# The routing of a fused attention and expert kernel: rounds two to five by order instead of by search

## The reference

```python
for t in range(S):
    state = f[:, :, t, :, None] * state + np.einsum('bhd,bhe->bhde', k[:, :, t], v[:, :, t])
    y[:, :, t] = np.einsum('bhd,bhde->bhe', q[:, :, t], state)
...
logits = x @ w_gate                       # 3072 tokens, 8 experts
order = np.argsort(-logits.flatten())
for idx in order:                         # best pair first
    tok, e = (int(idx) // E, int(idx) % E)
    if assigned[tok] >= 0 or counts[e] >= cap:
        continue
    assigned[tok] = e
    counts[e] += 1
for e in range(E):
    h = np.maximum(x[mask] @ w1[e], 0.0)  # 384 -> 1024
    out[mask] = h @ w2[e]                 # 1024 -> 384
...
h = x @ w_in                              # 384 -> 2048
g = h * np.clip(h + 3.0, 0.0, 6.0) / 6.0
out = g @ w_out                           # 2048 -> 384
```

## Time and profile before

| | us |
|---|---|
| median of 3 runs | 885.61 (885.39 to 890.78) |
| the profiled execution | 886.32 |
| its span | 883.8 |
| busy in it: TensorE, VectorE, ScalarE, GpSimd | 825.5, 384.3, 346.7, 324.8 |
| mean granted clock of TensorE | 0.964 |

### The profile page before, as it was taken

The page is one execution under the profiler, slowest core; times in us unless marked ns, Lnnn a source line. Parts: engine busy times, 40 slices in busy tenths (PEclk is TensorE's granted clock), DMA queues, the critical chain, the costliest instruction groups (busy, mean ns, idle before and its releaser), DMA issues.

```text
span 883.8 us, 15679 instructions
## 1 busy us (share of the span) xinstructions
PE 825.5 (93%) x6030; PEld 795.6 (90%) x6030; DVE 384.3 (43%) x717; ACT 346.7 (39%) x631; POOL 324.8 (37%) x249
## 2 busy tenths in 40 slices
PE   5999999965569999999999999999999999999995
PEld 4899989854459999999999999999999999999995
DVE  6778776556741442343143234324313322431331
ACT  4766766444521432333143233314323332432332
POOL 4676767634220522440161244116024422601001
PEclk8999999977679999999999999999999999999998
DMA  9999999322210221040121103012211200200000
GB/s 164 200 175 186 184 193 173 79 83 71 72 36 20 72 72 54 1 143 10 45 71 71 53 6 136 19 34 71 71 53 36 106 30 23 71 0 27 1 1 27
DMA packets 126806, 65.03 MB, mean 74 GB/s; under 512 B 102448, under 2 KB 119856, under 8 KB 126768
## 3 DMA queue, kind: packets, MB, share of 16 engines
q1 hardware_dynamic: 123696, 55.09, 28.8%
q0 software_dynamic: 3072, 9.44, 3.3%
HBM read 55.07 MB, written 9.44 MB: 73 GB/s over the span
## 4 chain that ended last, share of the span: by engine, by line
PE 89%; DVE 6%; issue 2%; SPq 1%; ACT 1%; DMA 1%; POOL 0%; DVEq 0%; POOLq 0%
PE psum L1580 23%; PE psum L1582 22%; PE psum L1581 22%; PE psum L1340 4%; PE psum L1392 3%; DVE junk L1179 3%; PE psum L1427 3%; PE psum L1442 2%; PE psum L1377 2%; PE psum L1506 2%; PE psum L1405 1%; PE psum L1435 1%; PE psum L1369 1%; SPq L499 1%; PE psum L1591 1%
## 5 line engine op out<-in xcount | busy, mean ns | idle before, releaser
L1322 DVE SCALAR_TENSOR_TENSOR psum<-rg,psum 128x384 f32<-128x384 f32 x128 | 72.0, 563 | 155.3 <-ACT rg L882 155.3
L882 ACT ACTIVATE rg<-psum,three 128x384 f32<-128x384 f32 x128 | 74.5, 582 | 153.1 <-PE psum L1582 153.1
L1580 PE MATMUL psum<-yh,w_high 128*128 128x384 f32 x384 | 130.7, 340 | 0.9
L1580 PE MATMUL psum<-w_high,gh 128*128 128x384 f32 x384 | 128.4, 334 | 0.3 <-DVE gl L1325 0.3
L1582 PE MATMUL psum<-yh,w_low 128*128 128x384 f32 x384 | 128.6, 335 | 0.0
L1581 PE MATMUL psum<-yl,w_high 128*128 128x384 f32 x384 | 128.5, 335 | 0.0
L1582 PE MATMUL psum<-w_high,gl 128*128 128x384 f32 x384 | 128.3, 334 | 0.0
L1581 PE MATMUL psum<-w_low,gh 128*128 128x384 f32 x384 | 128.3, 334 | 0.0
L716 POOL DMA_INDIRECT out_dram<-ys,ids x24 | 24.1, 1002 | 255.2 <-ACT ys L897 250.6
L1312 DVE SCALAR_TENSOR_TENSOR hl<-psum,hh 128x384 fp32r<-128x384 f32 x64 | 35.7, 558 | 166.2 <-ACT hh L872 166.2
L1325 DVE SCALAR_TENSOR_TENSOR gl<-psum,gh 128x384 fp32r<-128x384 f32 x128 | 71.4, 558 | 72.4 <-ACT gh L886 72.4
(11 more groups left out here) (191 smaller groups left out, 1616.1 us busy)
## 6 DMA issues: line engine op xcount, KB each, us to landing
raw<-in_moe_w_dram SPq DMA_DIRECT2D x16, 1536.0 KB, 6.5
f_in<-in_f_logit_dram SPq DMA_DIRECT2D x24, 192.0 KB, 4.6
k_in<-in_k_dram SPq DMA_DIRECT2D x24, 192.0 KB, 5.2
q_in<-in_q_dram SPq DMA_DIRECT2D x24, 192.0 KB, 5.5
v_in<-in_v_dram SPq DMA_DIRECT2D x24, 192.0 KB, 4.6
x_rows<-x_nat SPq DMA_DIRECT2D x24, 192.0 KB, 4.1
raw<-in_moe_w_in_dram SPq DMA_DIRECT2D x12, 256.0 KB, 4.3
raw<-in_moe_w_out_dram SPq DMA_DIRECT2D x12, 256.0 KB, 3.4
```

Source lines behind the costliest of these rows:

```text
L882: act.activation(rg[:, j % 2, :], banks[j % 3][:, 0:CAP], ACT.Relu, bias=three[:, 0:1]).then_inc(r_done, 1)
L1322: dve.scalar_tensor_tensor(out=bank, in0=rg[:, j % 2, :], scalar=6.0, in1=bank, op0=ALU.min, op1=ALU.mult).then_inc(gg_done, 1)
L1580: pe.matmul(bank, high, rhs_high, start=start, stop=False)
```

## The change

- `DIGITS` becomes `(2,)`: only the first round is searched, by two digits instead of three.
- Rounds two to five (`RANKED = 4`; before there were three more rounds, now there are four) find the threshold by order. `make_ranked` writes the negated logits of the applicants, and -1e38 for all others, into `vm_all`, 32 tiles of 8 (the last 8 tiles hold -1e38). TensorE turns them by four transposes into two equal copies of 128 lanes by 256 values, a lane being one of 16 groups of tiles and one expert. VectorE's `max` takes the 8 largest of each lane, a product with a 0/1 table (`lane_tile`) spreads them, and one matmul (`merged_ps`) puts the lists of the 16 lanes of an expert side by side, 128 values on 8 partitions; a second `max` takes the 8 largest, which are the 8 lowest applicants of the expert. Beside it ScalarE counts the applicants of each lane in the second copy (by the sum of signs), one matmul sums the lanes, and VectorE picks from the list by that number: an expert with 384 + k applicants gets the threshold that drops its k lowest, for k up to 7. So a round can drop at most 7 of an expert's applicants.
- TensorE's products of ones in the pauses of rounds two to five are gone; those of the first round are now 512 or 384 columns wide (`fill`).
- w1 of expert 0 is loaded as soon as the last chunk of the other weights is split, ahead of SyncE's waits for the rows of x. w2 of expert 0 gets a buffer of its own (`w2_raw`, in the place of w2l) and is loaded once the first round's values are turned. Its high part is made by ScalarE, two pieces in each of the rounds two to four, its low part by GpSimd.
- The first expert's start is in another order: `first_hidden(begin, end, j)` takes the first tile alone and the other two together, 256 columns wide; the second tile's transposes stand ahead of the first product; two warming products are gone.
- GpSimd's indirect DMAs take their bound from a register that is set once, and SyncE instead of GpSimd waits for the last stores.
- Six small tables more are made at the start by GpSimd and four small operations more by VectorE. In the exact scan that is jumped over, 12 steps that were written out are now a loop on VectorE and TensorE, so that its code is shorter.

```diff
-DIGITS = (3, 3, 4, 4)
-WINDOW = 1.0 / 16.0
-COARSE = len(DIGITS)
-BEFORE = tuple(sum(DIGITS[:r]) for r in range(COARSE + 1))
-COARSE_STEPS = BEFORE[COARSE]
+DIGITS = (2,)
+SEARCHED = len(DIGITS)
+RANKED = 4
+COARSE = SEARCHED + RANKED
+BEFORE = tuple(sum(DIGITS[:r]) for r in range(SEARCHED + 1))
+COARSE_STEPS = BEFORE[SEARCHED]
+LANE_TILES = 16
+RANKS = 8
+W2_ROUND = ((0, 2), (2, 4), (4, 6), (6, 6))
...
+            sp.wait_ge(chunk_split, NT)
+            sp.dma_start(raw[:, :].rearrange("p (a c n) -> p a c n", a=1, c=3),
+                         w1[0:1, :, :].rearrange("a (c p) n -> p a c n", p=P)).then_inc(raw_loaded, 16)
             for i in range(B):
                 sp.wait_ge(x_stored[i], 16 * TT)
...
             sp.sem_inc(x_rows_ready, 1)
-            weights(0)
+            sp.wait_ge(v_turned, 1)
+            sp.dma_start(w2_raw[:, :].rearrange("p (a g n) -> p a g n", a=1, n=DM),
+                         w2[0:1, :, :].rearrange("a (g p) n -> p a g n", p=P)).then_inc(w2_loaded, 16)
...
+            sp.wait_ge(stored, 48 * NE)
...
+            def finish_w2(i):
+                at = slice(3072 // PIECES * i, 3072 // PIECES * (i + 1))
+                pool.wait_ge(w2_high, i + 1)
+                pool.tensor_tensor(w2l[:, :, :].rearrange("p c n -> p (c n)")[:, at], w2_raw[:, at], w2h[:, :, :].rearrange("p c n -> p (c n)")[:, at].bitcast(F32),
+                                   ALU.subtract).then_inc(w2_low, 1)
             pool.wait_ge(x_rows_ready, 1)
-            expert_split(0)
+            split(0, w1h[:, :, :], w1l[:, :, :])
+            for i in range(PIECES):
+                finish_w2(i)
+            pool.wait_ge(w2_low, PIECES)
+            pool.sem_inc(split_done, 1)
...
+            act.wait_ge(rank_tables, 3)
+            for r in range(1, RANKED + 1):
+                act.wait_ge(ranked_turned_too, r)
+                act.activation(junk_a[:, 0:2 * P], ranked_too, ACT.Sign, scale=1.0, bias=half_big[:, 0:1],
+                               accum_out=lane_count[:, :]).then_inc(lane_counted, 1)
+                for i in range(*W2_ROUND[r - 1]):
+                    at = slice(3072 // PIECES * i, 3072 // PIECES * (i + 1))
+                    if i == 0:
+                        act.wait_ge(w2_loaded, 16)
+                    act.copy(w2h[:, :, :].rearrange("p c n -> p (c n)")[:, at],
+                             w2_raw[:, at]).then_inc(w2_high, 1)
...
+            def make_ranked(r):
+
+                dve.scalar_tensor_tensor(out=flat(vm[:, :, :]), in0=low_ps, scalar=-BIG, in1=flat(logit[:, :, :]),
+                                         op0=ALU.mult, op1=ALU.subtract).then_inc(ranked_made, 1)
+
+            def rank(r):
+
+                dve.wait_ge(ranked_turned, r)
+                dve.max(out=top_ps, in_=ranked_ps).then_inc(top_done, 1)
+                dve.wait_ge(top_done, r)
+                dve.tensor_tensor(spread[:, :].rearrange("p (n j) -> p n j", j=RANKS), top_ps.unsqueeze(1).broadcast_to([P, LANE_TILES, RANKS]),
+                                  lane_tile[:, :].unsqueeze(2).broadcast_to([P, LANE_TILES, RANKS]), ALU.mult).then_inc(spread_done, 1)
+                dve.wait_ge(merged, r)
+                dve.max(out=least_ps[:, 1:RANKS + 1], in_=merged_ps).then_inc(sorted_done, 1)
+                dve.wait_ge(lanes_summed, r)
+                dve.tensor_scalar(code_ps, lane_sum_ps, rank_code_at(RANKS - 1), rank_code_at(-1), ALU.min, ALU.max).then_inc(code_done, 1)
+                dve.wait_ge(code_done, r)
+                dve.wait_ge(sorted_done, r)
+                dve.scalar_tensor_tensor(out=picked[:, :], in0=rank_code[0:NE, :], scalar=code_ps, in1=least_ps, op0=ALU.is_equal,
+                                         op1=ALU.mult, accum_out=least[:, :]).then_inc(least_done, 1)
...
             measure()
             choose(0)
-            for r in range(COARSE):
+            for r in range(SEARCHED):
                 make_values(r)
-                if r == 0:
-                    set_scale()
-                else:
-                    set_window(r)
+                set_scale()
+                ranked_constants()
                 coarse(r)
+                limit_choice(r)
+                choose(r + 1)
+            dve.memset(least_ps[:, 0:1], BIG)
+            for r in range(1, RANKED + 1):
+                make_ranked(r)
+                rank(r)
                 limit_choice(r)
                 choose(r + 1)
             judge(COARSE)
...
+            def fill(bank, width, count):
+                rows_of_ones = ones_b[:, :].unsqueeze(1).broadcast_to([P, width // P, P])
+                for _ in range(count):
+                    pe.matmul(bank[:, 0:width], ones_b[:, :], rows_of_ones, start=True, stop=True)
+
+            def rank(r):
+                pe.wait_ge(ranked_made, r)
+                if r == 1:
+                    pe.wait_ge(rank_tables, 8)
+                pe.sem_inc(passed, 1)
+                for dst_ps, done in ((ranked_ps, ranked_turned), (ranked_too, ranked_turned_too)):
+                    for i in range(2):
+                        last = pe.transpose(dst_ps[:, P * i:P * i + P], vm_all[:, LANE_TILES * i:LANE_TILES * i + LANE_TILES, :].rearrange(
+                            "p n e -> p (n e)"), ident[:, :])
+                    last.then_inc(done, 1)
+                pe.wait_ge(spread_done, r)
+                pe.matmul(merged_ps, lane_expert[:, :], spread[:, :], start=True, stop=True).then_inc(merged, 1)
+                pe.wait_ge(lane_counted, r)
+                pe.matmul(lane_sum_ps, lane_expert[:, :], lane_count[:, :], start=True, stop=True).then_inc(lanes_summed, 1)
+                pe.wait_ge(least_done, r)
+                pe.matmul(thr_ps, least[:, 0:1].broadcast_to([NE, P]), minus[:, :], start=True, stop=True).then_inc(t_ready, 1)
+
             pe.wait_ge(x_copied, NT)
+            fill(p0, 4 * P, 2)
             pe.wait_ge(measured, 2)
             pe.matmul(peak_ps, peak[:, 0:1], ident[:, :], start=True, stop=True).then_inc(peak_turned, 1)
-            for r in range(COARSE):
+            fill(p0, 4 * P, 4)
+            for r in range(SEARCHED):
                 turn_values(r)
                 for i in range(DIGITS[r]):
-                    if i and i == DIGITS[r] - 1:
+                    if i:
                         pe.wait_ge(bits_ready, BEFORE[r] - r + i)
-                        for _ in range(16):
-                            pe.matmul(unread, ones_b[:, :], ones_b[:, :], start=True, stop=True)
+                    else:
+                        pe.wait_ge(scaled, 1)
+                    fill(p7, 3 * P, 8)
                     pe.wait_ge(ok_ready, BEFORE[r] + i + 1)
                     pe.matmul(digit_ps, above[:, :, :].rearrange("p a b -> p (a b)"), ok[:, :], start=True, stop=True).then_inc(n_ready, 1)
-                warm(2)
+                fill(p0, 4 * P, 1)
                 threshold(r)
-                if r < COARSE - 1:
-                    for wait, value in ((limited, 2 * r + 1), (limited, 2 * r + 2), (best_done, r + 2), (passed_over, r + 2)):
-                        warm(5)
-                        pe.wait_ge(wait, value)
-                        pe.sem_inc(passed, 1)
+            for r in range(1, RANKED + 1):
+                rank(r)
             count_choice(COARSE)
             def search(r):
...
+            def first_hidden(begin, end, j):
+                pe.wait_ge(xl_done, end)
+                at = slice(P * begin, P * end)
+                for c in range(3):
+                    last = product(banks[j][:, at], P * (end - begin), w1h[:, c, P * j:P * j + P], w1l[:, c, P * j:P * j + P], c,
+                                   xh[:, c, at], xl[:, c, at], c == 0, c == 2)
+                if end == 3:
+                    last.then_inc(h_ready, 1)
             first_turn(0)
-            warm_late(2)
-            pe.wait_ge(ids_known, 1)
-            pe.wait_ge(split_done, 2)
-            first_hidden(0)
             first_turn(1)
+            pe.wait_ge(split_done, 1)
+            first_hidden(0, 1, 0)
             first_turn(2)
-            first_hidden(1)
-            first_hidden(2)
+            first_hidden(0, 1, 1)
+            first_hidden(1, 3, 0)
+            first_hidden(1, 3, 1)
...
-                    pe.wait_ge(split_done, 2 + 2 * e)
+                pe.wait_ge(split_done, 2 + 2 * e)
```

177 lines of the change are left out of this document (106 added, 71 removed).

## The result

| | before | after |
|---|---|---|
| median | 886.5 (885.39 to 890.78, 4 runs) | 843.88 (843.52 to 844.19, 4 runs) |
| profiled execution, its span | 886.32, 883.8 | 844.1, 842.4 |
| mean granted clock | 0.964 | 0.977 |

The ratio is 0.9511 (95% interval 0.9478 to 0.9544).

A forecast was written before the change was run, and what follows sets the result against it. The prediction took TensorE to bound the expert stage and a chain of hand-overs the routing. Terms 2.6 + 0.8 + 27.8 + 3.1 = 34.3 us off 886.32 gave 852.0, as median 851.3; range 847 to 859 us.

The forecast's parts named there:

- a digit fewer: Round one: one search step goes, a gain of 2.61 us.
- ahead of round one: TensorE's late start behind the jump over the exact scan: gain 0.8 us, bounds 1.0 lost to 3.0 gained.
- rounds two to five: Values of round two to count of choices: four rounds at 5.5 us, gain 27.8 us, bounds 25.0 to 30.6.
- first expert: First expert's start to its third block: reordered and 256-wide products gain 3.1 us, bounds 1.5 and 3.6.
- gathers and stores by register: GpSimd's indirect DMAs: the register bound was taken as a gain of 0.
- the end: Stretch of 8.30 us behind the last copy: SyncE's last wait taken as 0, bounds 0 and 1.5 us gained.
- the chain: Routing ahead of the experts: no engine bounds it, hand-overs do, so time cut there shortens the run one for one.
- rival 1: Rounds two to five: `max` passes over the values once per result, 13.4 us in all, 864.7 us; 5 in 100.
- rival 3: Behind round five: `judge`'s flag stays up, exact rounds follow, 31.4 us each; one 882.7, two 914 us; 3 and 4 in 100.
- rival 4: First expert waits for w2 or w1, so the change misses the path; 856 us or so; no chance given.
- rival 2: First expert: the clock comes back later, 36 products at half clock cost 4 us, 855 us; 6 in 100.
- Start, gather, end: Ten more operations at the start, register bound and SyncE's last wait: 0, with up to 1.5 us gained at the end.

The follow-up runs named there:

- a_three_digits: The changed kernel with three digits instead of two in the first round; 846.83 us, ratio 0.952.
- the two scan runs: Kernel before with the jumped-over exact scan as a loop, 884.37 us, ratio 0.9966; changed kernel with the scan written out again, 847.96 us, ratio 0.9551.
- after_old_first_expert: The changed kernel with the first expert's hidden layer in the order of before and two late products of ones; 846.87 us, ratio 0.9531.
- a_number_as_bound: The changed kernel with the highest row of gathers and last stores as a number instead of a register; 845.84 us, ratio 0.9524.
- a_pool_waits: The changed kernel with GpSimd, not SyncE, waiting for the last stores; 845.99 us, ratio 0.9535.
- the moved buffers: Six kernels, three from the kernel before and three from the changed one, each with unused bytes shifting the attention stage's buffers; 884.64 to 887.1 and 844.08 to 846.05 us.
- a_moved_96_bytes: The changed kernel with 96 unused bytes ahead of the attention stage's buffers, so that input rows cross a multiple of 256; 846.05 us, ratio 0.9523.
- b_small_parts: The kernel before with the scan as a loop, the highest row in a register and SyncE waiting for the last stores; 884.38 us, ratio 0.9943.
- b_moved_864_bytes: The kernel before with 864 unused bytes ahead of x_nat, giving the attention stage's buffers their addresses in the changed kernel; 884.64 us, ratio 0.9952.

## Why the prediction was wrong

| term | forecast | measured | by |
|---|---|---|---|
| a digit fewer | 2.6 | 2.6 | `a_three_digits` |
| ahead of round one | 0.8 | 3.6 | the two scan runs (3.3 and 3.6) |
| rounds two to five | 27.8 | 28.0 | traces |
| first expert | 3.1 | 2.8 to 3.0 | `after_old_first_expert` |
| gathers and stores by register | 0 | 1.2 | `a_number_as_bound` |
| the end | 0 (to 1.5) | 1.7 | `a_pool_waits` |
| attention stage | no term | 1.2 | the moved buffers |

**Right: the chain.** Reading the routing as periods of a chain and pricing a new round from the nearest rows gave 5.5 us a round, against 5.30 to 5.56. The operation without a row was right too: `max` takes 0.45 us for 256 values and 0.30 for 128, so rival 1 fell. The Trainium skill ("Vector Engine (DVE) Microarchitecture Reference", "3.9 The match/index hardware and the swap-based sort pattern") has eight cells in series for it, and the trace agrees with one pass. The flag fell after four ranked rounds, so rival 3 fell. The first product waited for no weights: rival 4 fell. The clock was 1.00 from the first expert's first transposes (221.09) to its third block: rival 2 fell. More idle time did lower the mean clock of the rounds, from 0.67 to 0.56, but nearly every step had been priced at the lower level already, so that it cost nothing against the forecast. Against the upper level a round pays 0.25 us in its transposes (0.67 against 0.42).

**The step that failed most: "Ahead of round one".** The forecast took 0.8 "because the jump is still a jump", between bounds of a loss of 1.0 and a gain of 3.0. The runs showed a gain of 3.3 to 3.6, outside both: the mechanism (a shorter jump) was named and its size was wrong. TensorE's idle 2.16 us went whole, not in part, and with TensorE early the transposes follow the copies and run at the full clock, as the bound of 3.0 had assumed: together 2.5 us up to the first count. What neither the sum nor the bound had are VectorE's own jump (0.40 us) and the 0.40 us of the first search step, whose cause stays open. The last 0.2 us of the 3.6 lie at the end of round one, where the threshold's product takes 0.40 us (L1625) instead of 0.61 (L1521), at the upper clock level.

**"Start, gather, end".** Taken at 0 with a bound of 1.5 for the end. It was 1.7 for the end alone and 1.2 for the register. The register's 1.2 us are 0.68 at the first gather and 0.52 at the last stores. The stretch at the end was visible (8.30 us with idle engines), and so was the one from the list to its gather (1.16 us, in the rows above); the sum asked what hides such a stretch instead of what fills it.

**Attention.** That the ten more operations at the start lie beside the first loads and cost nothing was not contradicted by any trace. That new tables move every buffer behind them was not thought of. `a_moved_96_bytes` shows it as 1.5 us of stage.

**First expert.** 2.8 us from the first transposes to the third block instead of 3.1. The 18 products of 256 columns run 0.12 us apart as forecast, but from the first of them to the third block it is 2.60 us and not 2.2: the first product and the wait for the first hidden block's low part were not in the sum.

Together 2.8 + 2.9 + 1.2 us are nearly all of the 7.1 us that the span lost beyond the sum (41.4 to 34.3); 0.8 us more lies outside the span (2.5 us before, 1.7 after). Of that 0.3 us comes with the register (2.1 us with the bound as a number), nothing with the end's change (1.8 to 1.9 with GpSimd's wait), and the rest is open. The range failed because the small terms were thought to err to both sides, and those that missed by most erred to one. Even all of the forecast's own upper bounds together (2.6 + 3.0 + 30.6 + 3.6 + 1.5 us) give 844.3 us.

Open also is when the lower clock level comes into the first expert. It was seen in two of the seven profiles with the old order (`b_small_parts` and `b_moved_864_bytes`) and in none of the ten with the new one, which does not show that the new order is free of it. The other order of the weights' loads and splits is part of the change and was not tested by itself; the traces show no wait for it. No version that beats the changed kernel came out of the runs.

## What to carry to other kernels

A chain of hand-overs can be priced step by step from rows of other operations; here four rounds came to 27.96 us of gain for 27.8; the miss comes from what is off the chain. So go through the diff a second time for what changes without being meant: the length of code that engines jump over, the addresses of all buffers behind a new one, the form of an operand of a DMA, the engine that waits last, and what an engine off the path does at the moment at which the path now arrives. Where a row shows idle time by "issue", price its whole length as a bound of the gain, and more if the clock or a stream behind it depends on it.

## What the runs showed of the hardware

- Code that is only jumped over costs time: 2.16 to 2.45 us of idle TensorE and 0.4 of VectorE for a scan of twelve steps written out; as a loop neither is seen.
- Packets of 192 bytes took 15.3 to 15.4 ns on average where the rows of q, k and f in on-chip memory did not cross a multiple of 256 bytes, and 22.2 to 23.2 where they did.
- The first gather, an indirect DMA, started 1.15 us after the start of the list's copy with its bound as a number, and 0.48 with a register. The time outside the span was 2.1 us with the number, 1.7 to 1.9 without.
- The span ended 6.9 to 7.0 us after the last store's issue where GpSimd waited for it, 5.2 where SyncE did.
- Three copies of VectorE took 2.05 and 2.13 us where a subtraction of GpSimd ran beside them, and 0.90 where none did.
- TensorE busy 16.28 of 22 us, in blocks with pauses between them, was at a granted clock of 0.52.
